# Where the first weights begin within a partition: 32 bytes behind a multiple of 128

## Chip, cores and metric

The kernel runs on one core of one Trainium2 chip. The metric is the device time of one execution in microseconds, as the median of three runs.

## What is computed

The reference is a banded attention followed by two feed-forward layers on the same 2304 rows, all in float32:

```
q, k, v: (4, 8, 576, 64)          # batch, heads, sequence, head size
scores = q k^T / 8 - slope_h |i-j|, kept where 0 <= i-j < 128
x  = softmax(scores) v            # -> (2304, 512)
x  = gate1(x @ w_in1) @ w_out1    # 512 -> 2048 -> 512, g = h * sigmoid(1.702 h)
y  = gate2(x @ w_in2) @ w_out2    # the same sizes, g = clipped quadratic of h
```

## The kernel before

**Two parts.** The attention takes the first 138 us of the profile. The rest is the two feed-forward layers, cut into four phases (`PHASES`, u = 0 to 3; a layer is two phases, each with half of the hidden columns). A phase has an up part (`up_chunk`) and a down part (`down_chunk`), each in three chunks of 768 rows. Every block product is made from seven products (P1 to P7, a scheme of sums of quadrants), and each operand is split into a rounded high half and a low half, so a product takes three matmuls for each 128 rows of depth: high by high, high by low, low by high.

**Where the operands lie.** All operands of these matmuls lie in three tiles of SBUF. `arena` holds the seven operands made of the activations. The seven operands made of one weight block take a slot, and six slots are in use: slots 0 to 2 are the tile `w_first`, slots 3 to 5 are the tile `w_rest` (`w_place`: slot = w modulo 6). Weight blocks follow each other, so TensorE changes between the two tiles all the time.

**Which operand is stationary.** `multiply` (L1050 on) writes out the order of the matmuls. In the up parts one product of 6 matmuls takes all its weights from one block. In the down parts a product of 12 matmuls goes through four blocks, `8u + 4 + kt` with kt 0 to 3: in phase 0 these are in slots 4, 5, 0, 1, in phase 1 in slots 0, 1, 2, 3, in phase 2 in slots 2 to 5, in phase 3 in slots 4, 5, 0, 1. In both up and down parts the weights are the stationary operand (128 columns, loaded by LDWEIGHTS) and 384 columns of `arena` stream past, with one exception: in the down parts of phases 2 and 3 (`swapped`) a block of `arena` is stationary and 256 columns of weights stream past.

**What sets the order.** Each engine has its instructions in an order written out by hand, with counted semaphores between them. VectorE and ScalarE make the sums and the two halves of the operands (L1752, L1330 for `arena`; L1684, L1309 for weights), take the results out of PSUM and apply the gates; the SyncE queue moves operands, hidden values and weight blocks to and from device memory. In phases 2 and 3 some weight blocks are fetched ready made (`load_stock`).

**Addresses.** Tiles are laid one behind another in a partition, each beginning at a multiple of 32 bytes. In the compiled program of before `w_first` begins at byte 1152 (9 times 128), `arena` at 44160 (345 times 128), `raw_first` at 93312 (729 times 128), `wst` at 111744 (873 times 128), `half` (4 bytes) at 124032 (969 times 128). Because of the small tile `half`, `d1s` begins at 124064, and `w_rest` behind it at 130208, which is 1017 times 128 plus 32. Within `w_first`, `w_rest` and `arena` every matmul operand begins at a multiple of 512 bytes from the tile's start. So each weight operand in `w_first` and each operand in `arena` begins at a multiple of 128 bytes, and each in `w_rest` begins 32 bytes behind one.

Of the kernel before, what the change touches and what calls it, by code (L numbers as in the profile page):

```python
# [20 lines left out]
F32 = mybir.dt.float32  # L21
# [4 lines left out]
P = 128  # L26
# [86 lines left out]
def build(nc, qkT, v_main, v_tail, w_pairs, bias_table, identity, out):  # L113
# [3 lines left out]
    def sb(name, shape, dt, into=ctx):  # L117
        return into.enter_context(nc.sbuf_tensor(name, shape, dt))
# [11 lines left out]
    wd = nc.dram_tensor("wd", (len(STOCK), P, OPS, 2, 2 * P), F32, kind="Internal").ap()  # L130
    zd = nc.dram_tensor("zd", (TOKENS, D_MODEL), F32, kind="Internal").ap()

    w_first = sb("w_first", [P, 3, OPS, 2, 2 * P], F32R)
    arena = sb("arena", [P, ARENA * 4 * HALF], F32R)
    raw_first = sb("raw_first", [P, 3, 4 * HALF], F32)
    wst = sb("wst", [P, 12, 2 * P], F32)
# [1917 lines left out]
```

## Time and profile before

| | |
|---|---|
| median of three runs | 856.04 us (855.88 to 856.47) |
| span of the profiled execution, first to last instruction | 854.5 us |
| TensorE matmul busy | 847.2 us, 99% |
| TensorE weight load busy | 843.0 us, 99% |
| VectorE busy | 712.3 us, 83% |
| ScalarE busy | 538.6 us, 63% |
| granted TensorE clock | full over the span |

The profile shows one execution. Its span is its own time from the first instruction to the last; the 1.5 us between it and the median lie before and behind the instructions. Busy shares are of the span. In a timeline, matmuls of the same kind that follow each other are merged into one row with their count; the time from one row's start to the next row's start is what TensorE needed for that many matmuls, while the busy time of a row also holds the end of its last matmul, which runs beside the next one.

### The profile page before, as it was taken

The page shows a single profiled execution, that of the slowest core. Times are in us where ns is not written, and L with a number is a line of the kernel's source. Part 1 is how long each engine was busy: PE and PEld are TensorE (multiplying, and loading weights), DVE is VectorE, ACT ScalarE, POOL GpSimd, SP SyncE. Part 2 cuts the span into 40 slices and gives each one's busy share as a digit, 9 for nine tenths or more (in the row PEclk, how much of TensorE's full clock was granted, in tenths as well). Part 3 has the DMA queues.
Part 4 walks back from the last instruction along what each step waited for, and adds up shares of the span by engine and source line. Part 5 has one row for each costly group of instructions (what it writes and reads, how often), then busy time and mean ns, then how long its engine had stood idle before and what let it go on. Part 6 is the DMA issues. An engine that isn't in the chain of part 4 may idle for free.

```text
span 854.5 us, 15510 instructions
## 1 busy us (share of the span) xinstructions
PE 847.2 (99%) x5744; PEld 843.0 (99%) x5744; DVE 712.3 (83%) x982; ACT 538.6 (63%) x791; POOL 116.3 (14%) x82
## 2 busy tenths in 40 slices
PE   8999999999999999999999999999999999999998
PEld 7999999999999999999999999999999999999998
DVE  7888898786988966868988897989989788889784
ACT  7778786767765546768644456767465567665441
POOL 3788888000000000000000000000000000000000
PEclk9999999999999999999999999999999999999999
DMA  8988661767776337686764772687647643889722
GB/s 198 228 211 216 189 181 67 276 239 279 262 243 238 128 138 271 258 310 239 262 243 177 273 243 103 219 284 260 229 143 278 225 156 124 288 302 331 270 74 75
DMA packets 63257, 186.45 MB, mean 218 GB/s; under 512 B 7504, under 2 KB 14352, under 8 KB 59344
## 3 DMA queue, kind: packets, MB, share of 16 engines
q1 hardware_dynamic: 62896, 185.30, 63.6%
q8 instruction: 47, 0.77, 0.4%
q14 instruction: 26, 0.21, 0.1%
q10 hardware_dynamic: 288, 0.16, 0.1%
HBM read 113.09 MB, written 72.35 MB: 217 GB/s over the span
## 4 chain that ended last, share of the span: by engine, by line
PE 93%; DVE 3%; POOL 1%; DMA 1%; issue 1%; ACT 0%; SPq 0%; DVEq 0%; POOLq 0%
PE ps L1072 81%; PE ps L1040 5%; PE ps L1006 3%; PE ps L1019 3%; DMA raw_first<-yd 1%; POOL qk_hi L892 1%; PE ps L1034 1%; POOL k_lo L889 1%; PE ps L1049 1%; DVE probs L1642 1%; DVE qk_hi L1610 0%; DMA qk_raw<-qkT 0%; DVE arena L1752 0%; DVE qk_hi L1594 0%; ACT probs L1244 0%
## 5 line engine op out<-in xcount | busy, mean ns | idle before, releaser
L1072 PE MATMUL ps<-arena,w_first 128*128 128x384 f32 x1764 | 331.3, 336 | 0.0
L1072 PEld LDWEIGHTS ps<-arena,w_first 128*128 128x128 f32 x1764 | 310.7, 188 | 0.9 <-DVE arena L1752 0.5
L1072 PE MATMUL ps<-arena,w_rest 128*128 128x384 f32 x1260 | 240.4, 336 | 0.3 <-DVE ust L1855 0.3
L1072 PEld LDWEIGHTS ps<-arena,w_rest 128*128 128x128 f32 x1260 | 220.2, 188 | 0.8 <-DVE arena L1752 0.7
L1752 DVE TENSOR_TENSOR arena<-raw_first,arena 128x768 fp32r<-128x768 f32 (+1 forms) x114 | 148.9, 1319 | 77.1 <-ACT arena L1330 77.1
L1330 ACT ACTIVATE arena<-raw_first 128x768 fp32r<-128x768 f32 (+1 forms) x120 | 132.0, 1117 | 45.8 <-DVE raw_first L1711 38.8
L1072 PE MATMUL ps<-w_rest,arena 128*128 128x256 f32 x945 | 132.5, 281 | 0.0
L1072 PEld LDWEIGHTS ps<-w_rest,arena 128*128 128x128 f32 x945 | 121.1, 189 | 0.1
L1072 PE MATMUL ps<-w_first,arena 128*128 128x256 f32 x567 | 88.0, 282 | 0.0
L1752 DVE TENSOR_TENSOR arena<-raw_rest,arena 128x1536 fp32r<-128x1536 f32 (+1 forms) x48 | 71.4, 1487 | 8.6 <-ACT arena L1330 8.4
L1072 PEld LDWEIGHTS ps<-w_first,arena 128*128 128x128 f32 x567 | 76.0, 189 | 0.0
L1330 ACT ACTIVATE arena<-raw_rest 128x1536 fp32r<-128x1536 f32 (+1 forms) x48 | 60.9, 1268 | 23.0 <-PE ps L1072 21.0
L1376 ACT ACTIVATE d1s<-ps 128x384 f32<-128x384 f32 (+2 forms) x72 | 35.3, 490 | 40.9 <-PE ps L1072 40.9
L1244 ACT ACTIVATE probs<-probs,neg_max 128x256 f32<-128x256 f32 (+1 forms) x128 | 54.1, 472 | 6.5 <-DVE neg_max L1642 6.5
L1040 PE MATMUL ps<-v_sb,probs_t 128*128 128x65 f32 x448 | 57.1, 268 | 0.5 <-DVE heads_out L1655 0.5
L1040 PEld LDWEIGHTS ps<-v_sb,probs_t 128*128 128x128 f32 x448 | 55.3, 191 | 1.1 <-issue 0.9
L1642 DVE CUSTOM_DVE_ANT_0 probs<-ps,bias_sb 128x256 f32<-128x256 f32 (+1 forms) x128 | 44.6, 387 | 12.9 <-PE ps L1006 8.6
L1367 ACT ACTIVATE ps<-ps 128x384 f32<-128x384 f32 (+2 forms) x72 | 34.2, 476 | 30.1 <-PE ps L1072 28.9
L1674 DVE TENSOR_TENSOR wst<-wst 128x256 f32<-128x256 f32 (+1 forms) x90 | 48.5, 539 | 2.8
L1284 ACT ACTIVATE probs_t<-ps 128x512 f32<-128x512 f32 x64 | 37.8, 591 | 18.4 <-PE ps L1019 18.1
L1006 PE MATMUL ps<-qk_hi 128*128 128x256 f32 x158 | 47.6, 324 | 1.4 <-DVE qk_hi L1594 0.5
L892 POOL TENSOR_TENSOR qk_hi<-qk_raw,qk_hi 64x576 fp32r<-64x576 f32 x28 | 45.2, 1613 | 2.2
(125 smaller groups left out, 970.5 us busy)
## 6 DMA issues: line engine op xcount, KB each, us to landing
gd<-g SPq DMA_DIRECT2D x24, 1536.0 KB, 6.1
raw_rest<-gd SPq DMA_DIRECT2D x32, 768.0 KB, 5.1
wst<-w_pairs SPq DMA_DIRECT2D x32, 512.0 KB, 5.7
raw_first<-gd SPq DMA_DIRECT2D x16, 768.0 KB, 5.9
yd<-ust SPq DMA_DIRECT2D x6, 1536.0 KB, 6.3
qk_raw<-qkT SPq DMA_DIRECT2D x30, 288.0 KB, 4.1
wd<-ust SPq DMA_DIRECT2D x4, 1536.0 KB, 8.4
raw_first<-yd SPq DMA_DIRECT2D x4, 1536.0 KB, 7.7
```

What stands on the lines that cost most here:

```text
L892: nc.gpsimd.tensor_tensor(all_queries(qk_hi, head, LOWER), all_queries(qk_raw, head, UPPER), f32(all_queries(qk_hi, head, UPPER)), ALU.sub ...
L1006: last = nc.tensor.matmul(place, queries, k[:, key0:key0 + BAND], start=n_pass == 0 and (d > 0 or i == 0), stop=n_pass == 1 and (d > 0 or ...
L1040: last = nc.tensor.matmul(o_slot(2 * blk + e), probs_t[:, gi % 2, col:col + P], v_sb[:, h + e, max(blk - 1, 0) + piece], start=piece == 0, ...
L1072: last = nc.tensor.matmul(to, stationary, moving, start=start and n == 0, stop=n == len(steps) - 1, skip_group_check=True)
L1244: last = nc.scalar.activation(at, at, ACT.Exp, bias=neg_max[:, col:col + 1], scale=-1.0)
L1284: nc.scalar.activation(probs_t[:, gi % 2], pt_bank[gi % 2], ACT.Copy).then_inc(pt_copied[gi % 2], 1)
L1330: nc.scalar.activation(operand(k, i)[:, 0], source(k, i), ACT.Copy).then_inc(hi_made, 1)
L1367: nc.scalar.activation(b_bank(D, pos), a_bank(D, pos), ACT.Copy).then_inc(seeded_b, 1)
L1376: nc.scalar.activation(d1(D, pos), d_bank(D, pos), ACT.Copy).then_inc(d_copied, 1)
L1642: last = nc.vector.tensor_tensor_reduce(out=to[:, 0:width], in0=bank[:, i * BAND:i * BAND + width], in1=bias_sb[:, h + e, BAND - width:BAN ...
L1674: nc.vector.tensor_tensor(to, a, b, ALU.subtract).then_inc(w_added, 1)
L1752: nc.vector.tensor_tensor(at[:, 1], source(k, i), f32(at[:, 0]), ALU.subtract).then_inc(lo_made, 1)
```

## The change

Two unused tiles are laid in, one of 32 bytes ahead of `w_first` and one of 96 bytes ahead of `arena`:

```
+    sb("before_w_first", [P, 8], F32)
     w_first = sb("w_first", [P, 3, OPS, 2, 2 * P], F32R)
+    sb("before_arena", [P, 24], F32)
     arena = sb("arena", [P, ARENA * 4 * HALF], F32R)
     raw_first = sb("raw_first", [P, 3, 4 * HALF], F32)
     wst = sb("wst", [P, 12, 2 * P], F32)
```

No instruction is added, removed or moved. `w_first` begins at byte 1184, 32 bytes behind a multiple of 128, as `w_rest` does. `arena` begins at 44288, again a multiple of 128, and all tiles from `arena` on lie 128 bytes later than before.

## Rows read from the trace of the kernel before

**Rows 1.** The page: busy time and share of each engine, and the granted clock.

```profile
PE 847.2 (99%) x5744; PEld 843.0 (99%) x5744; DVE 712.3 (83%) x982; ACT 538.6 (63%) x791; POOL 116.3 (14%) x82
...
PEclk9999999999999999999999999999999999999999
```

**Rows 2.** Waits of TensorE: all of its waits in the feed-forward part.

```profile
PE ps L1072 <- DVE ust L1855: 0.3, 1, 0.3
```

**Rows 3.** Groups of instructions of the matmul line: busy us, mean ns of one.

```profile
L1072 PE MATMUL ps<-arena,w_first 128*128 128x384 f32 x1764 | 331.3, 336 | 0.0
...
L1072 PE MATMUL ps<-arena,w_rest 128*128 128x384 f32 x1260 | 240.4, 336 | 0.3 <-DVE ust L1855 0.3
```

**Rows 4.** Timeline of TensorE, phase 0 down: start, busy, instruction, count.

```profile
247.85 1.21 PE L1072 MATMUL ps<-arena,w_rest 128*128 128x384 f32 x6
248.90 1.23 PE L1072 MATMUL ps<-arena,w_first 128*128 128x384 f32 x6
249.96 1.21 PE L1072 MATMUL ps<-arena,w_rest 128*128 128x384 f32 x6
...
298.41 1.21 PE L1072 MATMUL ps<-arena,w_rest 128*128 128x384 f32 x6
```

**Rows 5.** Timeline of TensorE, phase 1 up: a long run within `w_rest`.

```profile
362.45 16.80 PE L1072 MATMUL ps<-arena,w_rest 128*128 128x384 f32 x96
379.09 1.23 PE L1072 MATMUL ps<-arena,w_first 128*128 128x384 f32 x6
```

**Rows 6.** Timeline of TensorE, phase 2 up: long runs in turn.

```profile
511.08 14.74 PE L1072 MATMUL ps<-arena,w_first 128*128 128x384 f32 x84
525.66 14.72 PE L1072 MATMUL ps<-arena,w_rest 128*128 128x384 f32 x84
540.23 14.74 PE L1072 MATMUL ps<-arena,w_first 128*128 128x384 f32 x84
```

**Rows 7.** Timeline of TensorE, phase 1 down, first and last row.

```profile
415.82 1.75 PE L1072 MATMUL ps<-arena,w_first 128*128 128x384 f32 x9
...
493.76 1.75 PE L1072 MATMUL ps<-arena,w_first 128*128 128x384 f32 x9
```

**Rows 8.** Timeline of TensorE, phase 2 down, first and last row.

```profile
584.31 1.22 PE L1072 MATMUL ps<-w_rest,arena 128*128 128x256 f32 x9
585.37 0.53 PE L1072 MATMUL ps<-w_first,arena 128*128 128x256 f32 x3
...
672.35 1.22 PE L1072 MATMUL ps<-w_rest,arena 128*128 128x256 f32 x9
```

**Rows 9.** Timeline of TensorE, phase 3 down, first and last row.

```profile
764.15 0.88 PE L1072 MATMUL ps<-w_rest,arena 128*128 128x256 f32 x6
764.87 0.88 PE L1072 MATMUL ps<-w_first,arena 128*128 128x256 f32 x6
...
849.89 0.88 PE L1072 MATMUL ps<-w_rest,arena 128*128 128x256 f32 x6
```

**Rows 10.** The chain that ended last: start, us, what.

```profile
148.43 330.76 PE ps L1072 x1890
480.06 8.54 DMA raw_first<-yd
...
497.32 354.17 PE ps L1072 x2514
```

**Rows 11.** Groups: making the weight operands, on ScalarE and VectorE.

```profile
L1684 DVE TENSOR_TENSOR w_first<-wst,w_first 128x1536 fp32r<-128x1536 f32 x12 | 21.1, 1755 | 3.1 <-ACT w_first L1309 2.7
...
L1684 DVE TENSOR_TENSOR w_rest<-wst,w_rest 128x1536 fp32r<-128x1536 f32 x12 | 21.0, 1754 | 2.1 <-ACT w_rest L1309 2.0
...
L1309 ACT ACTIVATE w_first<-wst 128x1536 fp32r<-128x1536 f32 x13 | 19.3, 1483 | 2.5 <-DVE wst L1674 2.5
L1309 ACT ACTIVATE w_rest<-wst 128x1536 fp32r<-128x1536 f32 x12 | 17.9, 1491 | 2.2 <-DVE wst L1674 2.2
```

**Rows 12.** DMA issues: count, KB each, median us to landing.

```profile
raw_first<-yd SPq DMA_DIRECT2D x4, 1536.0 KB, 7.7
w_first<-wd SPq DMA_DIRECT2D x21, 256.0 KB, 4.3
w_rest<-wd SPq DMA_DIRECT2D x21, 256.0 KB, 4.5
```

More of the change, by code:

```diff
@@ L131, in build @@
     zd = nc.dram_tensor("zd", (TOKENS, D_MODEL), F32, kind="Internal").ap()
+    sb("before_w_first", [P, 8], F32)
     w_first = sb("w_first", [P, 3, OPS, 2, 2 * P], F32R)
+    sb("before_arena", [P, 24], F32)
     arena = sb("arena", [P, ARENA * 4 * HALF], F32R)
```

## Prediction

> **What bounds the kernel.** I read the page first. TensorE is busy 99% of the span with matmuls and 99% with weight loads, at the full clock (2.4 GHz) throughout [rows 1]. The waits of TensorE come next: behind the attention there is one visible wait, of 0.3 us [rows 2]. So from 138 us on the time is the number of matmuls times their spacing, and an edit that moves only addresses can count only through that spacing. The groups don't show a difference between the two weight tiles: 336 ns for one matmul in either [rows 3]. But such a duration holds the end of the matmul, which runs beside the next one. What counts is the distance from start to start, and for this I read the timeline, where a row's start minus the next row's start gives it over many matmuls.
>
> **What the timeline shows.** A run of 96 matmuls within `w_rest` takes 379.09 - 362.45 = 16.64 us, which is 173.3 ns each [rows 5]. In the down part of phase 0, 12 matmuls make a cycle, 6 on `w_rest` and 6 on `w_first`. From 247.85 to 298.41 there are 24 cycles in 50.56 us: 2.107 us each, where 12 times 173.3 would be 2.080 [rows 4]. So a cycle costs 0.027 us more than its matmuls do in a long run. In phase 1 down the split is 9 on `w_first` and 3 on `w_rest`. From 415.82 to 493.76 there are 37 cycles in 77.94 us: again 2.107 us [rows 7]. Nine matmuls on `w_first` cost no more than six, so it isn't a dearer matmul on `w_first`. It is a price of each cycle, whatever its split, and so of changing tiles. In phase 2 up, 84 matmuls on one tile and 84 on the other take 540.23 - 511.08 = 29.15 us where 168 times 173.3 ns is 29.12: once more about 0.03 us for a pair of changes, with runs fourteen times as long [rows 6]. Which of the two changes pays shows in the rows as well, if less sharply: 84 on `w_first`, begun by the change from `w_rest`, take 14.58 us, and 84 on `w_rest` take 14.57, against 14.56 for 84 at 173.3 ns [rows 6]; in phase 0 the 6 on `w_first` have 1.06 us to themselves and the 6 on `w_rest` 1.05, against 1.04 [rows 4]. Most of it comes after the change to `w_first`, a smaller part at the last matmul ahead of it, while the first weights of `w_first` are being loaded. The way back costs next to nothing.
>
> **Why addresses may be behind it.** A change from `w_rest` to `w_first` is a change of the stationary operand's start from 32 bytes behind a multiple of 128 to a multiple of 128. Changes of slot within a tile are also jumps of many kilobytes, they occur all the time in the long runs, and they cost nothing [rows 5, 6]. Semaphores don't explain it either: in phase 0 down the change to `w_first` lies in the middle of a product, where TensorE waits for nothing, and long runs hold more than a dozen product starts for free. What the two tiles differ in is the start within 128 bytes and the place in the partition.
>
> **The change, step by step.** Nothing is added to any queue, so no wait is added, and nothing is queued behind one.
>
> 1. Stationary weights. The tile changes from `w_rest` to `w_first` are: 14 in each of the up parts of phases 0, 1 and 3, 3 in that of phase 2, and 42 (a change in each of 14 products of three chunks) in each of the down parts of phases 0 and 1. That is 129, three of which fall beside a short stall and don't show the price cleanly. If the price hangs on the start within 128 bytes, all changes become changes between like starts, and go at the spacing of [rows 5]: 126 times 0.027 us is 3.4 us. The bounds: nothing below, and 129 times 0.03, 3.9 us, above.
>
> 2. What of it is given back. Near 497 us TensorE waits [rows 2], and the chain of waits there runs through a transfer and VectorE from 480.06 to 497.32 [rows 10]. That stretch is released by work of TensorE just ahead of 480 and doesn't get shorter with it. Eight cycles of 2.107 us lie in it (17.3 us), so 7 or 8 prices of 0.027 us, 0.2 us, turn into a longer wait. What is late next is that load into `raw_first` and the sums behind it. 3.4 - 0.2 = 3.2 us remain. Elsewhere TensorE doesn't wait, and VectorE is busy 83% [rows 1], so 0.4% less time for it is small against its slack.
>
> 3. Streaming weights (phases 2 and 3, down). Here the moving operand changes its start. 62 cycles of 12 matmuls in phase 2, 3 of the 12 on `w_first`, take 672.35 - 584.31 = 88.04 us, 1.420 each [rows 8]. 60 cycles in phase 3, with 6 of 12 on `w_first`, take 849.89 - 764.15 = 85.74, 1.429 each [rows 9]. No run here stays within one tile, so the price of "all 32 behind" isn't in the trace. One bound is a line through the two: none on `w_first` would be 1.411, so with 63 cycles in each phase 63 x 0.009 + 63 x 0.018 = 1.7 us less. The other bound is that all cycles come to the dearer 1.429: 63 x 0.009 = 0.6 us more. I take the middle, 0.5 us less, as neither end is nearer to a row.
>
> 4. VectorE and ScalarE writing `w_first`: 1755 against 1754 ns and 1483 against 1491 ns for the same form on the two tiles [rows 11]. ScalarE at the new start would cost 13 x 8 ns, 0.1 us, all of it beside matmuls. I take nothing. Without that cover it would be 0.1 us.
>
> 5. Transfers. Into `w_first` 4.3 us, into `w_rest` 4.5 us at the median [rows 12]: at worst 0.2 us each, and they land well ahead of use, so nothing. The tiles from `arena` on move by a whole 128 bytes; `raw_first` goes from an odd multiple of 128 to an even one. Its loads from `yd` take 7.7 us [rows 12] and one is on the chain [rows 10]. The nearest rows that differ in the start are those of 4.3 and 4.5 us; 5% of 8.54 us is 0.4 us either way at one place, and in the sum I take nothing.
> The Trainium skill ("DMA: Bandwidth & Descriptors", How a descriptor splits into AXI transactions) says that a descriptor that begins off a multiple of 256 bytes also pays for the bytes from the multiple below. By that rule the loads into `raw_first` would be slightly cheaper after the change, an estimate of 4% of each (128 bytes on rows of 3072), and no row of before can show it.
>
> 6. Attention: all its tiles move by 128 bytes together and keep their start within 128. Nothing.
>
> **Sum.** 3.2 + 0.5 = 3.7 us. The span of 854.5 becomes 850.8, and the median of 856.04, 1.5 us above the span, becomes 852.3.
>
> **Rivals.**
> - *The start within 128 bytes doesn't matter, the change does nothing.* The price would then come from going back from the high end of the partition (130208 and up) to the low end (1152 and up). For it: the two tiles differ in this too, and the price has a direction. Against it: the way up is as far and is nearly free, and jumps within a tile of 14 kilobytes and more cost nothing [rows 5, 6]. The time is 856.0, 855.5 to 856.5. Chance 0.14.
> The Trainium skill ("TensorE: Matmul & The Clock Gate", Step-by-step: what each phase is for) speaks for this rival: it gives TensorE two independent read ports, so that loading the next weights takes nothing from the running matmul, and then where the weights begin can't matter. By it both the price of a change and the saving are zero. The trace doesn't agree fully, as 0.027 us for a pair of changes stands in [rows 4, 7].
> - *Part of it.* The changes keep some of their price, or the streaming phases turn to the dear end while the gain in step 1 is halved: 1.7 - 0.2 - 0.6 to 1.7 + 0.5, so 0.9 to 2.2 us, 853.8 to 855.1. Chance 0.07.
> - *Slower.* One mechanism: streaming weights that begin 32 bytes behind come out dear as soon as no aligned group stands between them. The dearest group of three in phase 2 is the one on `w_first`, 1.420 less the 1.06 of the nine on `w_rest` (585.37 - 584.31), 0.36 us; four such groups make a cycle of 1.440 [rows 8]. Against 1.420 and 1.429 that is 63 x 0.020 + 63 x 0.011 = 2.0 us more. It decides the sign only if step 1 pays less than 0.3 us, and it shows as slower from cycles of about 1.438 on. Against it: the nine on `w_rest` go at 0.118 us each and the three on `w_first` at 0.120, and the phase with more matmuls on the aligned tile is the slower one [rows 8, 9]. The time is 858.0, 857.7 to 858.4. Chance 0.05.
> - *The forecast's case*: 0.74. Its own range is 850.4 to 853.8: savings of 2.6 (3.2 less 0.6) to 5.3 us (3.6 plus 1.7), with 0.3 us on either side for runs that spread over 0.6.
>
> **The numbers.** 0.2% is 1.7 us, about what a measurement of this kernel tells from no change. Faster: 0.74 and most of "part of it", 0.79. Same: 0.16. Slower: 0.05. The range takes the likeliest case's own and reaches into "part of it": 850.3 to 855.3.
>
> **What would show it.** In the timeline after, phase 0 down should go at 2.080 us for 12 matmuls, and phase 1 down too: if both stay at 2.107, step 1 is wrong and the first rival right. In phases 2 and 3 down the cycle should take 1.41 to 1.43 us; 1.44 is the slow rival. The wait near 497 us should grow from 0.3 to about 0.5. Busy time of VectorE and ScalarE should stay within 0.2 us on the weight rows. What would make it wrong: the spacing within long runs is itself set by the weights' start, and the 173.3 ns of `w_rest` hold only because they alternate with `w_first`. Against this stand the 96 in a row.

## The result, and the profile after

The changed kernel takes 857.78 us (median of 14 runs, 857.22 to 858.83), the kernel before 855.99 us in the same session (14 runs, 855.88 to 856.47). The ratio is 1.0019, with a 95% interval of 1.0012 to 1.0027. It was to become 3.7 us faster; it became 1.8 us slower.

The page of the changed kernel: busy time of the engines.

```profile
span 855.7 us, 15510 instructions
...
PE 848.3 (99%) x5744; PEld 844.4 (99%) x5744; DVE 712.0 (83%) x982; ACT 538.6 (63%) x791; POOL 116.4 (14%) x82
```

TensorE is as full as before [rows 1], with the same instructions. It has 1.1 us more busy time and the span is 1.2 us longer. So the spacing of the matmuls changed. The timeline of the changed kernel (start, busy, instruction, count), phase 2 up, is to be held against [rows 6]:

```profile
512.24 15.00 PE L1074 MATMUL ps<-arena,w_first 128*128 128x384 f32 x84
527.07 14.72 PE L1074 MATMUL ps<-arena,w_rest 128*128 128x384 f32 x84
541.63 15.00 PE L1074 MATMUL ps<-arena,w_first 128*128 128x384 f32 x84
556.47 14.72 PE L1074 MATMUL ps<-arena,w_rest 128*128 128x384 f32 x84
```

A run of 84 on `w_rest` takes 14.56 us (541.63 - 527.07), 173.3 ns a matmul, as before. A run of 84 on `w_first` takes 14.83 and 14.84 us, 176.5 to 176.7 ns, where it was 14.58. Before, `w_first` was dearer only just after a change of tile. Now it is dearer at every matmul, by 3.3 ns, for as long as the run lasts.

Down parts of phases 0, 1, 2 and 3 in the changed kernel, first and last row of each:

```profile
247.73 1.22 PE L1074 MATMUL ps<-arena,w_first 128*128 128x384 f32 x6
...
298.37 1.22 PE L1074 MATMUL ps<-arena,w_first 128*128 128x384 f32 x6
...
417.04 1.75 PE L1074 MATMUL ps<-arena,w_first 128*128 128x384 f32 x9
...
495.23 1.75 PE L1074 MATMUL ps<-arena,w_first 128*128 128x384 f32 x9
...
586.23 1.21 PE L1074 MATMUL ps<-w_rest,arena 128*128 128x256 f32 x9
...
673.54 1.21 PE L1074 MATMUL ps<-w_rest,arena 128*128 128x256 f32 x9
...
764.04 0.87 PE L1074 MATMUL ps<-w_first,arena 128*128 128x256 f32 x6
...
794.72 0.94 PE L1074 MATMUL ps<-w_rest,arena 128*128 128x256 f32 x6 [0.28 <-DVE g L1857]
...
850.36 0.87 PE L1074 MATMUL ps<-w_first,arena 128*128 128x256 f32 x6
```

Twelve matmuls take 50.64 / 24 = 2.110 us in phase 0 (2.107 in [rows 4]), 78.19 / 37 = 2.113 in phase 1 (2.107 in [rows 7]), 87.31 / 62 = 1.408 in phase 2 (1.420 in [rows 8]), and 86.32 / 61 = 1.415 in phase 3 (1.429 in [rows 9]). The forecast had 2.080 for the first two and 1.41 to 1.43 for the others. The average of phase 3 holds the wait at 794.72; ahead of it and behind it twelve matmuls take 1.407 us. The one in [rows 9] also holds one longer cycle, near 792 us; elsewhere in that stretch twelve matmuls take 1.427.

By stages, from the starts of the rows at their borders:

| stage | before, us | changed, us | difference |
|---|---|---|---|
| from 138.6 to the down part of phase 2 | 445.3 | 447.2 | +1.9 |
| phase 2 down (weights stream) | 89.5 | 88.7 | -0.7 |
| phase 3 up | 87.9 | 88.75 | +0.9 |
| phase 3 down (weights stream) | 90.2 | 89.3 | -0.9 |

Where the weights are stationary 2.8 us were lost, where they stream 1.6 us were won. That leaves 1.1 of the span's 1.2 us (from unrounded differences).

### The profile page after: what moved, and what is told of

It reads as the page before. It is cut to its first block, busy times and chain, and to the rows that moved or that the text cites. A ratio compares the mean times of both kernels' runs of the same rounds, so it can differ in the third digit from the quotient of the medians.

```text
span 855.7 us, 15510 instructions
## 1 busy us (share of the span) xinstructions
PE 848.3 (99%) x5744; PEld 844.4 (99%) x5744; DVE 712.0 (83%) x982; ACT 538.6 (63%) x791; POOL 116.4 (14%) x82
## 4 chain that ended last, share of the span: by engine, by line
PE 91%; DVE 5%; POOL 1%; issue 1%; SPq 1%; DMA 0%; ACT 0%; DVEq 0%; POOLq 0%
PE ps L1074 79%; PE ps L1042 4%; PE ps L1008 3%; PE ps L1021 3%; DVE arena L1754 1%; POOL qk_hi L894 1%; PE ps L1036 1%; POOL k_lo L891 1%; PE ps L1051 1%; DVE probs L1644 1%; DMA qk_raw<-qkT 0%; DVE qk_hi L1612 0%; DVE raw_first L1713 0%; DVE g L1786 0%; DVE raw_first L1708 0%
## 5 line engine op out<-in xcount | busy, mean ns | idle before, releaser
L1409 ACT ACTIVATE g<-ps 128x384 f32<-128x384 f32 x48 | 23.4, 492 | 35.1 <-PE ps L1074 35.1
```

## The experiments

All move tiles only, except the last two, which repeat the changed kernel. They ran in four sessions, and the kernel before took 855.93 to 855.97 us in each, so medians can be compared across them. Ratios are to the kernel before. Positions are told as the distance of a weight tile's start from the start of `arena`, modulo 256 bytes. All operands begin at multiples of 512 bytes from their tile's start, so this is also the distance of any weight operand from any operand in `arena`. It is counted in the same way where `arena` is stationary and the weights stream. Before, it was 0 for `w_first` and 32 for `w_rest`; in the changed kernel 160 (1184 - 44288 = -43104) and 32.

**The arena alone.**

```
+    sb("before_arena", [P, 32], F32)
     arena = sb("arena", ...)
```

> w_first stays at byte 1152, the arena and all behind it move by 128 bytes (arena at an even multiple of 128, as in the changed kernel). In the changed kernel long runs on w_first go at 176.7 ns a matmul against 173.3 before and 173.3 on w_rest. Theory A (what counts is the distance of the weights' start from the arena's, taken within 256 or 512 bytes; it was 0 and 32 before, is 160 within 256 and 416 within 512 on w_first in the changed kernel): here the distance on w_first is 128 within 256 and 384 within 512, a value not seen yet, and w_rest keeps 32 and its 173.3 ns. Theory B (the arena's own place at an even multiple of 128 is dear for weights in the first tile): w_first at about 176.7 ns, time about 857.8 less what the streaming phases gain. Theory C (the weights' 32 bytes behind in w_first are dear by themselves): w_first at 173.3 ns as before, about 854 if the streaming phases keep the 2.0 us that they gained in the changed kernel.

Measured: 856.39 us, ratio 1.0004 (0.9995 to 1.0013). Long runs on `w_first` at 176.0 ns, the timeline of this kernel:

```profile
511.19 14.95 PE L1073 MATMUL ps<-arena,w_first 128*128 128x384 f32 x84
525.98 14.72 PE L1073 MATMUL ps<-arena,w_rest 128*128 128x384 f32 x84
540.54 14.95 PE L1073 MATMUL ps<-arena,w_first 128*128 128x384 f32 x84
```

14.79 us for 84 on `w_first`, which hasn't moved by a byte; 14.56 on `w_rest`. Theory C falls: `w_first` gets dearer without its 32 bytes. Theories A and B remain.

**The weights 32 bytes behind, the arena by 256 bytes.** It differs from the changed kernel by 128 bytes ahead of `arena`.

```
+    sb("before_w_first", [P, 8], F32)
     w_first = sb("w_first", ...)
+    sb("before_arena", [P, 56], F32)
     arena = sb("arena", ...)
```

> w_first 32 bytes behind as in the changed kernel, the arena and all behind it 256 bytes later than before (an odd multiple of 128 again). Distance of w_first from the arena: 32 within 256, 288 within 512. Theory A with a period of 256: w_first like w_rest, 173.3 ns in long runs and no price for a change of tile, 12 matmuls of phase 0 down at 2.080 us, 3.4 us less than before, so about 852.6. Theory A with a period of 512: not like w_rest, some other spacing. Theory B (the arena at an even multiple is dear): 173.3 ns on w_first. Theory C (32 behind is dear in w_first): 176.7 ns, about 857 to 858.

Measured: 850.66 us, ratio 0.9939 (0.9925 to 0.9952). What step 1 forecast for the change came true here. The timeline of this kernel, phase 2 up and phase 0 down:

```profile
508.07 14.72 PE L1074 MATMUL ps<-arena,w_first 128*128 128x384 f32 x84
522.63 14.72 PE L1074 MATMUL ps<-arena,w_rest 128*128 128x384 f32 x84
537.19 14.72 PE L1074 MATMUL ps<-arena,w_first 128*128 128x384 f32 x84
...
247.33 1.20 PE L1074 MATMUL ps<-arena,w_rest 128*128 128x384 f32 x6
...
297.25 1.20 PE L1074 MATMUL ps<-arena,w_rest 128*128 128x384 f32 x6
```

84 take 14.56 us on either tile. 24 cycles of twelve take 49.92 us, 2.080 each: the price for a change of tile is gone. The part up to phase 2 down takes 442.3 us where it took 445.3, and phase 3 up 87.5 where it took 87.9: 3.4 us less. Not all of it is the price: the profiled execution of before holds a wait of 0.3 us near 497 [rows 2], and this kernel has none there. Against the next kernel, which has the price of before and no such wait (445.0 and 87.9 us), 3.1 us are left, where step 1 had 3.4. The streaming phases give 88.2 and 89.1, which is 2.3 us less. Theory A with a period of 256 bytes holds, since the distance of `w_first` is 32 within 256 and 288 within 512.

**Everything by 128 bytes.**

```
+    sb("before_w_first", [P, 32], F32)
     w_first = sb("w_first", ...)
```

> All tiles, w_first too, move by 128 bytes; every distance between tiles is as before. Theory A: the spacing as before, 173.3 ns on both tiles with 0.027 us for a change of tile, phases 2 and 3 down at 1.420 and 1.429 us for 12, time 856.0. Theory B (the arena's own place): w_first at about 176.7 ns, about 858. Theory C: as before in the stationary phases. If phases 2 and 3 down come to 1.408 and 1.416 as in the changed kernel, their gain is from the arena's place and not from the distance.

Measured: 855.99 us, ratio 1.0000 (0.9991 to 1.0009). Twelve matmuls in phases 0 and 1 down at 2.107 us as before, phase 2 down 89.5 us. Theory B falls: `arena` lies where it does in the changed kernel and costs nothing. The run above speaks against theory C once more: `w_first` begins 32 bytes behind there, and its long runs go at 173.3 ns. This run also prices all that was moved along: attention tiles, `raw_first`, `wst` and the transfers into them, together nothing.

**The weights 32 bytes behind, the arena by 512 bytes** (`before_arena` of 120 words in place of 56).

> w_first 32 bytes behind, the arena and all behind it 512 bytes later than before. Distance of w_first from the arena: 32 within 256 and within 512, as that of w_rest. Theory A with either period: 173.3 ns on both tiles, no price for a change of tile, 12 matmuls of phase 0 down at 2.080 us, about 852.6. Theory B: 173.3 ns (the arena at an odd multiple). Theory C: 176.7 ns on w_first, 857 to 858.

Measured: 850.57 us, ratio 0.9940 (0.9928 to 0.9953), all stages within 0.1 us of those with 256 bytes.

**Both at distance 0.**

```
+    sb("before_w_rest", [P, 56], F32)
     w_rest = sb("w_rest", ...)
```

> w_rest is moved by 224 bytes, so that it too begins at distance 0 from the arena within 256 bytes, like w_first. Nothing else moves in the part ahead of it. If the price of a change of tile is that of going from distance 32 to distance 0, it is gone: 12 matmuls in phases 0 and 1 down at 2.080 us, 3.4 us less. If the price comes from going back to the low end of the partition, it stays at 2.107. In phases 2 and 3 down there is no row yet for distance 0 alone; where w_first had 6 in a row they ended at 120 ns each, so up to 1.440 us for 12. Time between 852.5 and 854.

Measured: 854.88 us, ratio 0.9988 (0.9979 to 0.9998). The timeline of this kernel, phase 0 down and phase 2 down:

```profile
247.42 1.20 PE L1073 MATMUL ps<-arena,w_rest 128*128 128x384 f32 x6
...
297.34 1.20 PE L1073 MATMUL ps<-arena,w_rest 128*128 128x384 f32 x6
...
582.50 0.52 PE L1073 MATMUL ps<-w_first,arena 128*128 128x256 f32 x3
582.86 1.24 PE L1073 MATMUL ps<-w_rest,arena 128*128 128x256 f32 x9
...
670.70 1.24 PE L1073 MATMUL ps<-w_rest,arena 128*128 128x256 f32 x9
```

49.92 / 24 = 2.080: no price for the change, though `w_rest` is still at the high end and `w_first` at the low end of the partition. So the price of before was that of going from distance 32 to 0, and the first rival's cause is excluded. With streaming weights this is the dearest kernel: 87.84 / 61 = 1.440 us for twelve.

**Other distances: 64 and 96, 192 and 224.** The same three pads in other sizes (in words: 16, 48 and 16; 48, 16 and 48, ahead of `w_first`, `arena` and `w_rest`).

> A look at other distances: w_first at 64, w_rest at 96 bytes from the arena within 256. Known so far, long runs with weights stationary: 173.3 ns at 0 and 32, 176.0 at 128, 176.7 at 160. If the spacing only depends on the distance of that tile, each of the two has a spacing of its own here, in long runs of both, probably 173 to 177. A rival: the two good values belong to the lower half of the 256 bytes, then both 173.3 and at most a price for changes, time 851 to 856.

> The rest of the circle: w_first at 192, w_rest at 224 bytes from the arena within 256. By the lower-half rival both are dear, 176 to 177 ns in long runs, about 3 ns x 3024 matmuls = 8 to 10 us more than the best, 859 to 861. If the spacing is smooth around 0, then 224 is near 173.3 and 192 between.

Measured: 856.14 us, ratio 1.0002 (0.9993 to 1.0012), and 856.14 us, ratio 1.0003 (0.9994 to 1.0013). Timelines of phase 2 up, first of 64 and 96:

```profile
510.07 14.72 PE L1075 MATMUL ps<-arena,w_first 128*128 128x384 f32 x84
524.63 14.73 PE L1075 MATMUL ps<-arena,w_rest 128*128 128x384 f32 x84
539.20 14.83 PE L1075 MATMUL ps<-arena,w_first 128*128 128x384 f32 x84
553.87 14.72 PE L1075 MATMUL ps<-arena,w_rest 128*128 128x384 f32 x84
```

then of 192 and 224:

```profile
511.46 14.73 PE L1075 MATMUL ps<-arena,w_first 128*128 128x384 f32 x84
526.03 15.00 PE L1075 MATMUL ps<-arena,w_rest 128*128 128x384 f32 x84
540.86 14.73 PE L1075 MATMUL ps<-arena,w_first 128*128 128x384 f32 x84
```

At 192 a run takes 14.57 us, at 224 14.83. The lower-half rival and the smooth one both fall. `w_rest`, free so far, is as dear as `w_first` was as soon as its distance is 224. And at 64 the same tile takes 14.56 us in one run and 14.67 in the next. So it is at 96: in phase 1 up of this kernel 90 matmuls on `w_rest` go at 176.7 ns, from 332.94 us on, and the 96 from 362.45 us on at 173.4. With streaming weights 96 is as dear as 0: the matmuls on `w_rest` in phase 3 down go at 120.0 ns.

**The weights unmoved, both at 32.**

```
+    sb("before_arena", [P, 56], F32)
     arena = sb("arena", ...)
```

> w_first stays at byte 1152, a multiple of 128; the arena and all behind it move by 224 bytes, so the arena begins 96 bytes behind a multiple of 128 and both weight tiles are at distance 32 from it. If only the distance counts (theory A): as in the kernels with the weights 32 behind and the arena at an odd multiple, 173.3 ns in all long runs, 2.080 us for 12 in phases 0 and 1 down, 1.400 and 1.413 in phases 2 and 3 down, 850.6 us. If the starts within 128 or 256 bytes count by themselves, some of these numbers differ, and the time lies nearer 856 or above.

Measured: 850.95 us, ratio 0.9941 (0.9926 to 0.9956). The gain comes without moving the weights at all. Up to the end of phase 3 up each border agrees with the 256 byte kernel within 0.02 us; phase 3 down takes 89.6 us instead of 89.1. Both kernels have a wait of 0.5 us there, near 788 us, and twelve matmuls take 1.400 us ahead of it in both. Behind it they take 1.413 here and 1.400 there.

**Both at 16, both at 48.** Here the offset is within the weight tiles (`w_first` 4 words, `w_rest` 60; and 12 and 4), as in

```
-    w_first = sb("w_first", [P, 3, OPS, 2, 2 * P], F32R)
+    w_first = sb("w_first", [P, 4 + 3 * OPS * 4 * P], F32R)[:, 4:].rearrange(...)
+    sb("before_arena", [P, 56], F32)
```

> Both weight tiles at distance 16 from the arena within 256 bytes (by an offset within the tiles). Known: 0 and 32 give 173.3 ns in long runs and no price for a change between like distances; with weights streaming, 12 matmuls take 1.440 us at 0 and 1.400 at 32 in phase 2 down. If the step between those two lies on a grid of 32 bytes, 16 behaves like one of them, 1.440 or 1.400; if it is gradual, about 1.42. Time 850.6 to 855.

> Both weight tiles at distance 48. Known: 32 gives 173.3 ns, 64 gave 174.7 ns in most long runs. On a grid of 32 bytes: like 32, 850.6. Gradual: 174 ns in long runs, 2 us more. A lower time than at 32 would need the streaming phases below 1.400 us for 12.

Measured: 857.50 us (855.25 to 859.69), ratio 1.0022 (1.0007 to 1.0036), and 852.54 us, ratio 0.9960 (0.9945 to 0.9975). At 48 the stationary phases are as at 32 and the streaming ones dearer (89.5 us in phase 2 down against 88.2). That is 1.420 us for twelve at 48. At 16 it is 1.424, near the 1.42 that the gradual theory had for streaming weights. With stationary weights neither theory fits at 16. Two stretches of its timeline in one execution:

```profile
512.86 15.00 PE L1073 MATMUL ps<-arena,w_first 128*128 128x384 f32 x84
527.70 15.00 PE L1073 MATMUL ps<-arena,w_rest 128*128 128x384 f32 x84
...
705.01 16.80 PE L1073 MATMUL ps<-arena,w_first 128*128 128x384 f32 x96
721.65 1.20 PE L1073 MATMUL ps<-arena,w_rest 128*128 128x384 f32 x6
```

First 14.84 us for 84 matmuls, 176.7 ns each; later 16.64 for 96, 173.3 ns each. Same addresses, two spacings: the long runs go at 176.7 ns in the up parts of phases 0 and 2 and at 173.3 in those of phases 1 and 3. This may also be behind the wide spread of its times, which isn't shown, as one execution alone was profiled.

**Both at 160.** The changed kernel with `w_rest` moved to the distance that `w_first` has.

```
+    sb("before_w_first", [P, 8], F32)
     w_first = sb("w_first", ...)
+    sb("before_arena", [P, 24], F32)
     arena = sb("arena", ...)
+    sb("before_w_rest", [P, 32], F32)
     w_rest = sb("w_rest", ...)
```

> The changed kernel with w_rest moved by 128 bytes, so that both weight tiles are at distance 160, which in the changed kernel only w_first has. If the distance sets the spacing, w_rest goes from 173.3 to 176.7 ns as w_first does: all 3024 matmuls with stationary weights at 176.7, 12 in phases 0 and 1 down at 2.120 us, 3024 x 3.33 ns = 10.1 us more than with both at 32 (850.6), so about 860 to 862. If it is the tile w_first or its place that is dear, w_rest stays at 173.3 and the time near 857.8.

Measured: 862.06 us, ratio 1.0069 (1.0054 to 1.0084). The timeline of this kernel, phase 2 up:

```profile
514.33 15.00 PE L1075 MATMUL ps<-arena,w_first 128*128 128x384 f32 x84
529.17 15.00 PE L1075 MATMUL ps<-arena,w_rest 128*128 128x384 f32 x84
544.01 15.00 PE L1075 MATMUL ps<-arena,w_first 128*128 128x384 f32 x84
```

14.84 us on either tile. Against both at 32 (850.66) the whole costs 11.4 us. 7.5 of them lie ahead of phase 2 down (449.9 against 442.3 us), 1.5 in phase 3 up (89.0 against 87.5), so 9.0 in the stationary phases where 10.1 was worked out ahead, and 1.5 and 1.0 in the two streaming ones. The distance sets the spacing of `w_rest` as it does that of `w_first`.

**Both at 192** (pads of 48, 16 and 40 words).

> Both weight tiles at distance 192, where w_first alone had 173.3 ns in long runs. With like distances no price for a change: 2.080 us for 12 in phases 0 and 1 down. With weights streaming the three on w_first took 351 ns there in half of the cycles, so 12 at 1.40 to 1.43 us. Time 850.5 to 853. If the neighbouring dear values (160 and 224) show that 192 is only good by luck of the order, long runs come out above 173.3.

Measured: 849.90 us, ratio 0.9937 (0.9920 to 0.9953), the lowest median of all, not separable from both at 32. Stationary phases at 173.3 ns throughout. Phase 3 down of this kernel holds the stretch to look at:

```profile
763.01 0.87 PE L1075 MATMUL ps<-w_rest,arena 128*128 128x256 f32 x6
...
787.04 0.87 PE L1075 MATMUL ps<-w_rest,arena 128*128 128x256 f32 x6
787.75 0.87 PE L1075 MATMUL ps<-w_first,arena 128*128 128x256 f32 x6
788.81 0.94 PE L1075 MATMUL ps<-w_rest,arena 128*128 128x256 f32 x6 [0.20 <-DVE g L1858]
...
790.26 0.84 PE L1075 MATMUL ps<-w_rest,arena 128*128 128x256 f32 x6
...
843.30 0.84 PE L1075 MATMUL ps<-w_rest,arena 128*128 128x256 f32 x6
```

Ahead of the wait twelve matmuls take 24.03 / 17 = 1.414 us, behind it 53.04 / 39 = 1.360. From a stall of 0.2 us on, the spacing of all that follows is another, and a shorter one. One of the four executions of this kernel took 852.0 us, the others 849.8 to 849.9. As an estimate, 39 cycles at 1.414 instead of 1.360 are 2.1 us, so that one may have kept the longer spacing; it wasn't profiled.

**Distance 160 without the weights' 32 bytes.**

```
+    sb("before_arena", [P, 24], F32)
     arena = sb("arena", ...)
```

> The mirror of the run with the arena 224 bytes later: w_first stays at byte 1152, a multiple of 128, and only the arena and what is behind it move, by 96 bytes, so that w_first is at distance 160 and w_rest at 32, the distances of the changed kernel. If the distance is all that counts: w_first at 176.7 ns in long runs, w_rest at 173.3, 12 matmuls in phases 0 and 1 down at 2.110 and 2.113 us, time 857.2 to 858.5. If the weights' 32 bytes behind had a part in the loss, it is nearer 856.

Measured: 857.42 us, ratio 1.0016 (1.0007 to 1.0026). Long runs on `w_first` 14.84 us, on `w_rest` 14.56. The start 32 bytes behind has no part in the loss.

**The changed kernel twice more**, one execution each, without an edit.

> The changed kernel once more. Its runs spread over 1.6 us (857.2 to 858.8) where those of the kernel before spread over 0.6, and its profiled run explains 1.2 of the 1.8 us. If the same addresses can settle at more than one spacing, entered by chance at a stall, another execution shows another spacing in some stage, with the span different by up to 1 us. If the spacing is fixed, the stages are the same within 0.1 us and the spread lies in the attention or in waits.

> The same as the run before it: a third execution of the changed kernel in the profile, read in the same way.

Measured: 858.04 and 857.21 us. All stages agree within 0.2 us with the first profile of this kernel, except phase 3 down. The rows of the first of the two, then of the second:

```profile
763.35 0.86 PE L1074 MATMUL ps<-w_rest,arena 128*128 128x256 f32 x6
...
792.89 0.86 PE L1074 MATMUL ps<-w_rest,arena 128*128 128x256 f32 x6
...
794.73 0.95 PE L1074 MATMUL ps<-w_rest,arena 128*128 128x256 f32 x6 [0.27 <-DVE g L1857]
...
796.23 0.87 PE L1074 MATMUL ps<-w_rest,arena 128*128 128x256 f32 x6
...
851.61 0.86 PE L1074 MATMUL ps<-w_rest,arena 128*128 128x256 f32 x6
```

```profile
763.01 0.86 PE L1074 MATMUL ps<-w_rest,arena 128*128 128x256 f32 x6
...
792.55 0.86 PE L1074 MATMUL ps<-w_rest,arena 128*128 128x256 f32 x6
...
795.88 0.86 PE L1074 MATMUL ps<-w_rest,arena 128*128 128x256 f32 x6
...
850.74 0.86 PE L1074 MATMUL ps<-w_rest,arena 128*128 128x256 f32 x6
```

Ahead of the wait 21 cycles take 29.54 us in both, 1.407 each. Behind it 39 cycles take 55.38 us in one, 1.420 each, and 54.86 in the other, 1.407 each: 0.5 us in all. So the same program goes on at one spacing or another from the wait on. The profiled execution of the result had the shorter one, the kernel with the arena 96 bytes later the longer one.

A visible wait near 790 us stands in the profiles of eight kernels and repeats. In four of them the spacing turns there (the first repeat, the arena 96 and 224 bytes later, both at 192), in four it stays (the changed kernel, its second repeat, the arena by 256 and by 512 bytes). What decides it isn't known. Nor is how often each comes. The medians differ by 0.6 us more than the profiled spans do; the longer spacing can cover a part of this, and the wait of 0.3 us near 497, which the profile of before holds and that of the changed kernel doesn't, another part.

All of it in one table. The ns are start to start in the runs of 84 of phase 2 up, on `w_first` and `w_rest`. A run on `w_first` begun by a change from distance 32 to 0 holds the price of the change, 0.02 us or 0.3 ns a matmul. Then the length of phase 2 down.

| kernel | distances | long runs, ns | phase 2 down, us | median, us |
|---|---|---|---|---|
| before | 0, 32 | 173.6, 173.3 to 173.5 | 89.5 | 855.99 |
| changed | 160, 32 | 176.7, 173.3 | 88.7 | 857.78 |
| arena alone | 128, 32 | 176.0, 173.3 | 88.6 | 856.39 |
| arena 256 or 512 | 32, 32 | 173.3, 173.3 | 88.2 | 850.66, 850.57 |
| all by 128 | 0, 32 | 173.6, 173.3 | 89.5 | 855.99 |
| both 0 | 0, 0 | 173.3, 173.3 | 90.7 | 854.88 |
| 64 and 96 | 64, 96 | 173.3 or 174.6, 173.3 to 173.5 (in phase 1 also 176.7) | 90.3 | 856.14 |
| 192 and 224 | 192, 224 | 173.5, 176.5 | 89.3 | 856.14 |
| weights unmoved | 32, 32 | 173.3, 173.3 | 88.2 | 850.95 |
| both 16 | 16, 16 | 176.7, 176.7 (phases 1 and 3: 173.3) | 89.7 | 857.50 |
| both 48 | 48, 48 | 173.3, 173.3 | 89.5 | 852.54 |
| both 160 | 160, 160 | 176.7, 176.7 | 89.7 | 862.06 |
| both 192 | 192, 192 | 173.3, 173.3 | 89.0 | 849.90 |
| arena 96 | 160, 32 | 176.7, 173.3 | 88.7 | 857.42 |

## Why the prediction was wrong

**What bounds the kernel** was read rightly: TensorE's spacing, and nothing else. Every kernel here differs from the first in addresses only, and they span 12 us.

**Step 1 failed, at its condition "if the price hangs on the start within 128 bytes, all changes become changes between like starts".** The price of before was real and was removed by like distances, as the kernels with both at 32 and both at 0 show, and its size was nearly right (3.1 us, where step 1 had 3.4). But what has to be alike is the distance from the arena's start within 256 bytes, and within 128 bytes the two aren't told apart. The change moved `w_first` by 32 and `arena` by 128, so the distance went from 0 to 160, not to 32. In the changed kernel the price of a change of tile is replaced by 3.3 ns at every matmul on `w_first` in a long run, and by cycles of 2.110 and 2.113 us. The 128 bytes of `arena` were taken for neutral because its start stayed a multiple of 128. The rows of before couldn't show the period: they hold the distances 0 and 32 alone. That was no ground to give the case 0.74. The text's own doubt, that long runs depend on the weights' start, was set aside with the run of 96 on `w_rest`, which shows distance 32 and says nothing of 160.

**Step 2**, the part given back near 497 us, wasn't put to the test in the changed kernel, whose TensorE came later there: its one visible wait in the feed-forward part is that in phase 3. But it fails in the kernel with the arena 256 bytes later. There TensorE comes 3 us earlier, and it has no wait near 497 at all. The kernel with everything 128 bytes later has none either, at the spacing of before. So that wait isn't a fixed part of the program, and nothing was given back there. Both have a start-to-start distance of 0.3 to 0.4 us at that place, where before has 0.6.

**Step 3** was right in sign and too small: 0.5 us less forecast, 1.6 measured, at the far bound of 1.7. That the bound held is luck. It was worked out for `w_first` at 32, which gives 1.400 in phase 2 and not 1.411, and the changed kernel has it at 160. Distance 0 is dear for streaming weights (1.440 for twelve with both there), and `w_first` left it. Leaving it isn't enough by itself: with 64 and 96 phase 2 down takes 90.3 us, more than before.

**Steps 4 to 6** held as far as the time goes. VectorE and ScalarE write `w_first` in 1754 and 1483 ns (1755 and 1483 in [rows 11]), as the groups of the changed kernel show:

```profile
L1686 DVE TENSOR_TENSOR w_first<-wst,w_first 128x1536 fp32r<-128x1536 f32 x12 | 21.1, 1754 | 3.2 <-ACT w_first L1311 3.1
...
L1311 ACT ACTIVATE w_first<-wst 128x1536 fp32r<-128x1536 f32 x13 | 19.3, 1483 | 2.6 <-DVE wst L1676 2.6
```

The kernel with everything 128 bytes later takes the time of before, so the moved transfers are worth nothing. Loads from `yd` into `raw_first` take 7.0 us at the median in the changed kernel and 7.5 in that one, where the tile begins at an even multiple of 128 bytes, against 7.7 in [rows 12]. But with the arena 256 bytes later it begins at an odd multiple again, and they take 6.5. So no run here shows the effect that was estimated for them from the Trainium skill ("DMA: Bandwidth & Descriptors", How a descriptor splits into AXI transactions): the medians of four loads go up and down by more than 4% whichever multiple the tile begins at. Loads into `w_rest` take 5.2 us in the changed kernel, 0.7 more than in [rows 12] where step 5 had at most 0.2, and TensorE has no wait behind them.

**The rivals.** None had this mechanism. "Slower" put the loss in the streaming phases, where in fact time was gained. The first rival's cause, going back to the low end of the partition, is excluded by both at 0. That addresses don't matter at all is refuted too: both at 160 against both at 32 is 11.4 us with the same instructions. The rule beside it (the Trainium skill, "TensorE: Matmul & The Clock Gate", Step-by-step: what each phase is for), by which loading the next weights takes nothing from the running matmul, doesn't agree with these runs as far as the time goes: the spacing depends on where the two operands lie towards each other.

## What to carry to other kernels

Where matmuls bound the time, the distance between the stationary and the moving operand is a parameter of its own. Here the best placement takes 6 us less than before, 0.7%, and the worst 6 us more. It is free to try by an unused tile. Fit a rule of placement to more than two positions before relying on it; two positions can't tell a period of 128 from one of 256, nor an absolute start from a distance. And read start to start over long runs: the mean duration of one matmul hid the price of a change in the kernel before (336 ns in both rows of [rows 3]).

## What was not expected of the hardware

- The spacing of matmuls of 384 streaming columns with 128 stationary ones, all fp32r, is in long runs 173.3 ns at distances 0, 32, 48 and 192, 176.0 at 128, 176.7 at 160, 176.6 at 224. The order has no simple shape. Of 256 columns it is 120.0 ns at 0 and 116.7 at 32 (phase 2 down).
- Moving every tile together by 128 bytes changes nothing (855.99 us); adding 256 bytes to a distance changes nothing (850.66 and 850.57).
- At some distances there are two steady spacings for the same addresses: 173.3 and 176.7 ns at 16, 173.3 and 174.7 at 64, 173.4 and 176.7 at 96. For streaming weights, twelve take 1.414 or 1.360 us at 192, 1.407 or 1.420 with 160 and 32, and 1.400 or 1.413 with both at 32 (there in two kernels with the same distances and other addresses). In these three cases of streaming weights a wait of 0.2 to 0.5 us lies at the point where it turns.
- What keeps this state, and why the distance counts at all, stays open, as does whether a placed stall could choose the shorter spacing. The runs change addresses alone and show the spacing, not what goes on behind it.
